# Halving the row scans at the start of an mLSTM and mixture-of-experts kernel

## The reference, cut to what matters

```python
for t in range(S):
    m_new = np.maximum(f_gate[:, :, t] + m, i_gate[:, :, t])
    f_stab = np.exp(f_gate[:, :, t] + m - m_new)
    i_stab = np.exp(i_gate[:, :, t] - m_new)
    m = m_new
    C = f_stab[..., None, None] * C + i_stab[..., None, None] * np.einsum('bhd,bhe->bhde', vt, kt)
    n = f_stab[:, :, None] * n + i_stab[:, :, None] * kt
    h_tilde = np.einsum('bhde,bhe->bhd', C, qt)
    denom = np.maximum(np.abs(np.einsum('bhd,bhd->bh', n, qt)[:, :, None]), 1.0)
    y[:, :, t] = sigmoid(o_gate[:, :, t]) * h_tilde / denom
```

## Time and profile before

| | us |
|---|---|
| median of 3 runs | 825.75 |
| lowest, highest | 824.54, 826.11 |
| the profiled execution | 824.76 |
| its span in the trace | 823.0 |
| first tile's exponent product starts | 17.80 |
| last product of the mixer starts | 177.29 |

### The profile page before, as it was taken

How to read it: one execution, slowest core, us unless ns; L and a number is a source line. 1 busy time by engine, 2 the same in 40 slices (tenths; PEclk the granted TensorE clock), 3 DMA queues, 4 the chain that set the end, 5 groups by cost and what they waited for, 6 DMA issues and landing times.

```text
span 823.0 us, 17685 instructions
## 1 busy us (share of the span) xinstructions
PE 782.3 (95%) x6036; PEld 726.4 (88%) x6036; DVE 521.2 (63%) x1424; ACT 468.7 (57%) x997; POOL 394.0 (48%) x467
## 2 busy tenths in 40 slices
PE   5899999989989999999999999999999999999994
PEld 4898898977878889999999989999998999999894
DVE  5566777767669667765865686487658657442431
ACT  5455545522427752884587287538826762892672
POOL 3545455454623752655166246507633651673233
PEclk9999999999999999999999999999999999999998
DMA  4999999714420312121121212112121212121000
GB/s 75 140 157 167 152 183 154 137 57 119 123 60 20 86 49 69 48 72 46 48 79 49 69 37 66 56 46 71 49 81 30 61 49 70 53 67 40 2 1 24
DMA packets 137987, 60.96 MB, mean 74 GB/s; under 512 B 104696, under 2 KB 136184, under 8 KB 137912
## 3 DMA queue, kind: packets, MB, share of 16 engines
q1 hardware_dynamic: 135608, 52.13, 29.8%
q0 software_dynamic: 2304, 7.87, 3.0%
HBM read 51.67 MB, written 8.26 MB: 73 GB/s over the span
## 4 chain that ended last, share of the span: by engine, by line
PE 63%; DVE 6%; ACT 5%; issue 2%; POOL 1%; DMA 0%; ACTq 0%; POOLq 0%
PE bank L1857 7%; PE bank L1942 7%; PE bank L1858 6%; PE bank L1860 6%; PE bank L1944 6%; PE bank L1943 6%; PE bank L1862 3%; PE bank L1861 3%; PE bank L1898 3%; PE bank L1900 3%; PE bank L1899 3%; PE bank L1794 2%; PE bank L1886 1%; PE bank L1883 1%; DVE unit L1535 1%
## 5 line engine op out<-in xcount | busy, mean ns | idle before, releaser
L1272 POOL TENSOR_TENSOR gl_lo<-unit,gl_hi 128x384 fp32r<-128x384 f32 x128 | 130.5, 1019 | 263.2 <-ACT gl_hi L1732 263.1
L1942 PE MATMUL bank<-Wo_hi,gl_hi 128*128 128x320 f32 x384 | 124.8, 325 | 0.5 <-POOL gl_lo L1272 0.5
L1944 PE MATMUL bank<-Wo_hi,gl_lo 128*128 128x320 f32 x384 | 118.6, 309 | 0.0
L1943 PE MATMUL bank<-Wo_lo,gl_hi 128*128 128x320 f32 x384 | 118.4, 308 | 0.0
L1532 DVE SCALAR_TENSOR_TENSOR unit<-bank,unit 128x384 f32<-128x384 f32 x104 | 57.8, 556 | 74.7 <-ACT bank L1725 74.7
L1696 ACT ACTIVATE hid_hi<-bank 128x384 fp32r<-128x384 f32 x64 | 31.5, 491 | 125.6 <-PE bank L1862 125.6
L1713 ACT ACTIVATE unit<-bank 128x384 f32<-128x384 f32 x128 | 62.3, 487 | 50.4 <-PE bank L1862 41.3
L1857 PE MATMUL bank<-x_hi,Wi_hi 128*128 128x384 f32 x224 | 80.2, 358 | 2.4 <-DVE unit L1535 1.6
L1858 PE MATMUL bank<-x_hi,Wi_lo 128*128 128x384 f32 x224 | 75.8, 338 | 0.0
L1942 PEld LDWEIGHTS bank<-Wo_hi,gl_hi 128*128 128x128 f32 x384 | 72.5, 189 | 3.1 <-POOL gl_lo L1272 3.1
L1535 DVE TENSOR_TENSOR unit<-unit,bank 128x384 f32<-128x384 f32 x128 | 70.9, 554 | 4.4
(11 more groups left out here) (296 smaller groups left out, 2084.0 us busy)
## 6 DMA issues: line engine op xcount, KB each, us to landing
stage<-in_moe_w_dram SPq DMA_DIRECT2D x32, 320.0 KB, 3.0
stage<-in_moe_w_dram SPq DMA_DIRECT2D x32, 256.0 KB, 2.6
stage<-in_moe_w_dram SPq DMA_DIRECT2D x96, 64.0 KB, 2.4
k_in<-in_k_dram SPq DMA_DIRECT2D x24, 160.0 KB, 3.8
q_in<-in_q_dram SPq DMA_DIRECT2D x24, 160.0 KB, 4.5
o_in<-in_o_gate_dram SPq DMA_DIRECT2D x24, 160.0 KB, 4.0
v_in<-in_v_dram SPq DMA_DIRECT2D x24, 160.0 KB, 3.6
x_rows<-xt SPq DMA_DIRECT2D x24, 160.0 KB, 3.2
```

Source lines behind the costliest of these rows:

```text
L1272: nc.gpsimd.tensor_tensor(gl_lo[:, b, :], ex[:, b, :], gl_hi[:, b, :].bitcast(F32), ALU.subtract).then_inc(gl_ok, 1)
L1942: nc.tensor.matmul(acc[j][:, 0:DM], gl_hi[:, f % RG, t_], Wo_hi[:, f, :], start=(f == 0), stop=False)
L1943: nc.tensor.matmul(acc[j][:, 0:DM], gl_hi[:, f % RG, t_], Wo_lo[:, f, :], start=False, stop=False)
L1944: ins = nc.tensor.matmul(acc[j][:, 0:DM], gl_lo[:, f % RG, t_], Wo_hi[:, f, :], start=False, stop=(f == NF2 - 1))
```

## The change

Five things are changed, all in the prologue and the first tiles.

1. The DVE steps on rows are done twice, for columns 0 to 383 (three chunks) and then for 384 to 767 (`rows_of(0)`, `rows_of(1)`). The second half's maximum starts from the first half's last column. The low parts of the second half are put off until after tile 0's product of scores and W (`low_parts(1)` in DVE's `body`).
2. PE's turning into columns and ACT's exponentials are done by halves as well: the first half before tile 0, the second half inside tile 1 (`columns_of_rows(1)` between `addend` and `products`, `by_token(1)` at the end of ACT's tile 1), in bank 7. PE, POOL and DVE wait for them (`cols_step` 6) where they first use chunk 3, or the bank. ACT's high parts of the second half come after tile 0's W.
3. SP's loads no longer wait for the pads: tile 0's k, q, o follow the gates at once, v waits for its own clearing, and k and q of tile 1 follow. Six loads are issued ahead of the exponents' rows. `part_rows` is written after the first weight piece, and `load_exponents(0, 1)` comes after tile 3's loads.
4. Two small DMAs (`first_rows` of the low parts) go from SP to ACT, and the three of `w_gate` go to GpSimd's queue.
5. POOL clears `exp_l[0]` and the v buffers first; ACT prepares its constants by halves; PE starts its constant products when `ident` is there, 21 of them instead of 18.

```diff
-            sp.wait_ge(const_ok, 3)
             load(0, 0, 0)
+            sp.wait_ge(values_zero, 1)
             load_values(0, 0, 0)
-            sp.wait_ge(exp_const, 1)
+            load_rows(0, 1, 1)
+            sp.wait_ge(exp_const, 2)
             sp.wait_ge(parts_hi, 1)
-            first_rows(0)
+            first_rows(sp, 0)
             sp.wait_ge(parts_hi, 2)
             first_columns(0)
-            sp.wait_ge(rows_step, 10)
-            first_rows(1)
-            sp.wait_ge(rows_step, 11)
+            sp.wait_ge(rows_step, C_LO)
             first_columns(1)
-            sp.dma_start(part_rows.rearrange("j r t -> r j t"), parts[:].bitcast(F32)).then_inc(parts_out, 16)
-            load(0, 1, 1)
+            load_out_gates(0, 1, 1)
+            sp.wait_ge(values_zero, 3)
             load_values(0, 1, 1)
-            for n, (a, w) in enumerate(XK):
-                sp.dma_start(wg[0:w, n, 0:E], w_gate[a:a + w, :]).then_inc(wg_in, 16)
             load(0, 2, 2)
             load_values(0, 2, 2)
-            sp.wait_ge(parts_out, 16)
-            load_exponents(0, 1)
...
             weights(0)
+            sp.wait_ge(rows_step, ALL_ROWS)
+            sp.dma_start(part_rows.rearrange("j r t -> r j t"), parts[:].bitcast(F32)).then_inc(parts_out, 16)
...
             for j in range(NCH - RING):
                 turn(j, (0, j), 0, RING + j, j % RING)
+                if j == 0:
+                    sp.wait_ge(exp_const, 4)
+                    sp.wait_ge(parts_out, 16)
+                    load_exponents(0, 1)
...
+            pool.wait_ge(wg_zero, 1)
+            for n, (a, w) in enumerate(XK):
+                nc.gpsimd.dma_start(wg[0:w, n, 0:E], w_gate[a:a + w, :]).then_inc(wg_in, 16)
...
+            def low_parts(half):
+                mine, first = slice(half * SPAN, (half + 1) * SPAN), half * HALF_STEPS
+                dve.wait_ge(parts_hi, 2 * half + 1)
+                row_step(nc.vector.tensor_tensor(parts[:, 1, mine], A_rows[:, mine], parts[:, 0, mine].bitcast(F32), ALU.subtract))
+                dve.wait_ge(rows_step, first + C_AT)
+                dve.wait_ge(parts_hi, 2 * half + 2)
+                row_step(nc.vector.tensor_tensor(parts[:, 3, mine], c_rows[:, mine], parts[:, 2, mine].bitcast(F32), ALU.subtract))
...
+            rows_of(0)
+            rows_of(1)
...
                 if last:
                     finish(*last)
+                if peeled(b) and b == 0 and c == 0:
+                    low_parts(1)
...
+            row_constants(0)
+            column_constants(0)
+            row_constants(1)
+            high_parts(0)
+            column_constants(1)
+            act.wait_ge(rows_step, A_LO)
+            first_rows(act, 1)
+            by_token(0)
...
                     nc.scalar.activation(W[u][:, par], pE[par], ACT.Exp).then_inc(w_ok, 1)
+                if peeled(b) and b == 0 and c == 0:
+                    high_parts(1)
...
+                if peeled(b) and b == 0 and c == 1:
+                    by_token(1)
...
-            pe.wait_ge(const_ok, 3)
-            warm(18)
-            pe.wait_ge(rows_step, 13)
...
+            pe.wait_ge(const_ok, 1)
+            warm(21)
+            columns_of_rows(0)
             warm(7)
             pe.wait_ge(cols_ok, 1)
             pe.wait_ge(cols_step, 3)
-            pe.wait_ge(exp_const, 1)
-            pe.wait_ge(pads_ok, 2 * RING)
+            pe.wait_ge(exp_const, 2)
+            pe.wait_ge(pads_ok, 2 * RING + 1)
...
                 if last:
                     carried(*last)
                     addend(*last)
+                if peeled(b) and b == 0 and c == 1:
+                    columns_of_rows(1)
                 if last:
                     products(*last)
```

More of the change, by code:

```diff
@@ L217, in peeled, with own_half, first_rows @@
             return isinstance(g, int)
+        FIRST_STEPS, HALF_STEPS = 3, 10
+        A_AT, C_AT, A_LO, C_LO = (FIRST_STEPS + n for n in (5, 6, 7, 8))
+        LAST_AT = FIRST_STEPS + 10, FIRST_STEPS + HALF_STEPS + 8
+        ALL_ROWS = FIRST_STEPS + 2 * HALF_STEPS
+        def own_half(b, c):
+            return peeled(b) and b == 0 and c == RING
         def three_beside(g, u):
             return u == RING - 1 and not (peeled(g) and g < RING)
+        def first_rows(eng, j):
+            for par in range(2):
+                row = par * DP + H + j
+                eng.dma_start(exp_r[0][row:row + 1, :, :].bitcast(F32),
+                              parts[par:H:2, j, 0:SPAN].bitcast(F32)).then_inc(exp_in[0], 16)
         @block.sync
@@ L342, in _ @@
                                         pattern=[[-1, NP]], channel_multiplier=1).then_inc(const_ok if n == 3 else pool_step, 1)
+            nc.gpsimd.memset(exp_l[0][:].bitcast(F32), 0.0).then_inc(exp_zero, 1)
+            for u in range(RING):
+                nc.gpsimd.memset(v_in[u][:], 0.0).then_inc(values_zero, 1)
             for u in range(RING):
@@ L364, in body @@
                 g, u, i = tile_of(b, c)
+                if own_half(b, c):
+                    pool.wait_ge(cols_step, 6)
                 if c < NCH - 1:
@@ L501, in body @@
                 last = before_it(b, c, 1)
+                if own_half(b, c):
+                    dve.wait_ge(cols_step, 6)
                 if last:
@@ L549, in _, with row_constants, column_constants @@
             act.wait_ge(const_ok, 2)
-            for half in range(2):
-                nc.scalar.copy(exp_r[half][:, :, :], head_sel[:, :].unsqueeze(2).broadcast_to([P, NP, SPAN]))
-            act.wait_ge(exp_zero, 2)
-            for half in range(2):
+            def row_constants(half):
+                nc.scalar.copy(exp_r[half][:, :, :], head_sel[:, :].unsqueeze(2).broadcast_to([P, NP, SPAN])).then_inc(exp_const, 1)
+            def column_constants(half):
+                act.wait_ge(exp_zero, half + 1)
                 for mine in HALVES:
@@ L565, in _ @@
-            nc.scalar.activation(eZ[:, :, :].rearrange("p (b c) h -> p b c h", b=B),
-                                 pcols[1].rearrange("p c (b h) -> p b c h", b=B), ACT.Exp)
-            for par in range(2):
-                rows = slice(par * 64, par * 64 + 64)
-                nc.scalar.activation(carry[rows, :, :].rearrange("p (b c) n -> p b c n", b=B),
-                                     plast[rows, :].rearrange("p (b n r c) -> p r b c n", b=B, r=2, c=NCH)[:, par],
-                                     ACT.Exp).then_inc(cols_step, 1)
+                ins.then_inc(exp_const, 1)
@@ new lines, in high_parts, with by_token @@
+            def high_parts(half):
+                mine, first = slice(half * SPAN, (half + 1) * SPAN), half * HALF_STEPS
+                act.wait_ge(rows_step, first + A_AT)
+                nc.scalar.copy(parts[:, 0, mine], A_rows[:, mine]).then_inc(parts_hi, 1)
+                act.wait_ge(rows_step, first + C_AT)
+                nc.scalar.copy(parts[:, 2, mine], c_rows[:, mine]).then_inc(parts_hi, 1)
+            def by_token(half):
+                chunks = slice(half * RING, (half + 1) * RING)
+                act.wait_ge(prepT, half + 1)
+                nc.scalar.activation(eA[:, :, :].rearrange("p (b c) h -> p b c h", b=B)[:, :, chunks],
+                                     pcols[half][0].rearrange("p (c b h) -> p b c h", b=B, h=H), ACT.Exp).then_inc(cols_step, 1)
+                nc.scalar.activation(eZ[:, :, :].rearrange("p (b c) h -> p b c h", b=B)[:, :, chunks],
+                                     pcols[half][1].rearrange("p (c b h) -> p b c h", b=B, h=H), ACT.Exp)
+                for par in range(2):
+                    rows = slice(par * 64, par * 64 + 64)
+                    nc.scalar.activation(carry[rows, :, :].rearrange("p (b c) n -> p b c n", b=B)[:, :, chunks],
+                                         plast[half][rows, :].rearrange("p (b n r c) -> p r b c n", b=B, r=2, c=RING)[:, par],
+                                         ACT.Exp).then_inc(cols_step, 1)
@@ L692, in carried @@
                     pe.wait_ge(fin_step, g * 6 - 4)
+                if peeled(g) and g == 1:
+                    pe.wait_ge(cols_step, 6)
                 pe.wait_ge(c_ok, states_through(b, c - 1))
```

111 lines of the change are left out of this document (55 added, 56 removed).

## The result

The changed kernel takes 821.82 us, median of 8 runs (820.15 to 824.64); the kernel before takes 826.25 in the same comparison. The ratio is 0.9944, 95% interval 0.9923 to 0.9965, so 4.6 us are won (4.4 by the two medians), and between 2.9 and 6.4. Forecast were 819.6 and 6.0 us. Two later comparisons of the same kernel gave 0.9903 (0.9868 to 0.9938) and 0.9928 (0.9895 to 0.996).

A forecast was written before the change was run, and what follows sets the result against it. PE bounds the steady run from tile 4, so time won before it is kept: 6.1 us by tile 2, less 1.2 for the clock, plus 1.1 at tile 3, is 6.0; 825.75 - 6.0 = 819.75, forecast 819.6, range 817.6 to 822.8.

The forecast's parts named there:

- The steady run decides, and keeps what is won ahead of it: Mixer from tile 4: PE busy 120.73 of 122.17 us, so each us won before should be won at the end.
- Tile 0 opens behind DVE's second half, at 14.3: Prologue: PE waits for DVE's row steps on both halves; opening at 14.3 against 17.80, bounds 13.7 and 15.2.
- Cover for the small DMAs, 1.6 us: Prologue: the last small exponent DMA lands at 12.7, 1.6 us before tile 0 opens.
- Moved DMAs cost and bring nothing: Prologue: DMAs on other queues save only issue time; no gain counted, gate-weight DMAs on POOL costed at nothing.
- Tiles 0 and 1 in 3.16 and 6.05: First tiles: tile 0 takes 3.16; tile 1 takes 4.8 plus 0.65 for second-half columns and 0.6 waiting for ACT.
- 1.2 for the clock: Tiles 0 and 1: one stretch of PE at half clock, charged 1.2 us, bounds 0 and 1.6.
- the forecast's case: Whole kernel: one half-clock stretch in tiles 0 and 1, 6.0 us gained, 818.8 to 820.8 us, chance 0.50.
- the rival of two or more stretches: Prologue: a second half-clock stretch costs another 1.2 to 1.6 us; part of a rival at 821 to 823, chance 0.22.
- Tile 3 loses its 1.10: Tile 3: its load is issued at 21 to 22 instead of 32.06, so its extra 1.10 us goes.
- The rest unchanged: After the first tiles: the steady pace and the experts stay as they were.
- gain lost later: Kernel's end: it waits for something not moving with the tiles, such as a DMA; within 1.6 of 825.75, chance 0.06.
- less is won: Prologue: two half-clock stretches, DVE at its upper bound, or exponents' rows behind six loads; 821 to 823 us, chance 0.22.

The follow-up runs named there:

- early loads alone: Kernel before, with tile 0's k, q, o loaded at once and tile 1's k and q issued ahead of the small DMAs; 824.15 us, ratio 0.9958.
- early clearing: Changed kernel with the two memsets PE waits for moved ahead, behind the third step of DVE's second half; 819.40 us, ratio 0.991 to before.
- more constant products: Changed kernel with 26 and 15 constant products instead of 21 and 7 around the first half's transposes; 819.84 us, ratio 0.9904 to before.
- both: Changed kernel with early clearing and 24 and 9 constant products, run twice; 819.35 and 819.32 us, ratios 0.9888 and 0.9894 to before.
- columns by GpSimd: Kernel of both, with the last two small exponent DMAs issued by GpSimd and 7 constant products before tile 0, not 9; 818.81 us, ratio 0.9882.

## Why the prediction was right, step by step

- **The steady run decides, and keeps what is won ahead of it.** Right. From tile 4 to the experts' start the changed kernel takes 135.39 us (173.87 - 38.48), before it took 136.08 (178.91 - 42.83). The 0.7 less was not forecast; all three profiles have it (135.38 to 135.42), and early loads alone doesn't (136.07). Its cause stays open. The mixer's last product starts at 172.25, 170.98 and 171.42, where 171.3 was forecast.
- **Tile 0 opens behind DVE's second half, at 14.3.** Right: 14.16, 14.19 and 14.49. A scan of 384 took 0.94 to 1.00 (0.95 was taken), a plain step 0.55 with a start to start of 0.47 to 0.58 (0.50), the diagonal 0.24 (0.35). The early clearing showed that this was the wait.
- **Cover for the small DMAs, 1.6 us.** They had landed by 13.02 or earlier, as the early clearing showed, so the cover was 1.1 us or a little more.
- **Moved DMAs cost and bring nothing.** Right for this kernel, by the run with all of them on SP. Behind the early clearing it is not: there two small DMAs moved from SP to GpSimd are issued by 10.83 instead of 11.65, and tile 0 opens 0.8 us sooner.
- **Tiles 0 and 1 in 3.16 and 6.05, and 1.2 for the clock.** The tiles at full clock take 3.15 and 6.44: the second was 0.4 short, by two errors. PE's own work was put at 5.45 and is 6.11, the wait for ACT at 0.6 and is 0.33. The clock is the term that was mis-sized: 1.2 us was charged, for one stretch, with bounds of 0 and 1.6. The first profile lost 2.6 us in three stretches. There the clock fell at 11.4, before the hole ahead of tile 0 had begun, while the prediction had it fall after that hole; PE had been idle from 7.92 to 9.35 as well, and that hole was not counted. Two other executions had the one stretch, in the place forecast (between 14 and 19), which cost 1.3 and 1.4 by the same sum, and tile 4 at 37.22 and 37.62, 5.6 and 5.2 us ahead, where 6.0 was forecast. So the forecast's case and the rival of two or more stretches both occur, from one execution of the same program to the next. The hole before the transposes isn't the same in them: 1.43 us in the first, 0.86 and 0.92 in the others, whose first constant products took longer (see the last section). Whether that decides is not shown.
- **Tile 3 loses its 1.10.** Right in all three: its load was issued at 22.50, it took 6.06.
- **The rest unchanged.** The work is, its time is not, for two reasons. The first is the clock. Behind tile 4, the last microseconds left out, the changed kernel's profiles had two stretches at half clock each, of 3.4 or 6.8 us, which cost 1.4 to 1.9 us each (the leads before and behind them). So had most other variants, near 168 to 181, 227 to 237, or 266 to 274, while three profiles (more constant products, early loads alone, and the second of both) had none. The kernel before had none there in its profile at a clock of 0.994, but its other 50 runs have a mean of 0.9904, so stretches are common there too.
- **The gain kept to the end.** Only in part, and this is the second reason. The prediction gave "gain lost later" 0.06 and thought of a DMA. What the trace shows are three short DVE steps in the experts' first token lists (`sel`, `mem`, `lo`) that end only with POOL's product beside them. Taken together they are over their shortest times (0.22, 0.24 and 0.18) by 0.6 us before, by 2.3, 2.0 and 2.2 in the changed kernel's profiles, by 1.2 with more constant products, 0.5 with the early clearing, 1.0 and 1.7 with both, and 0.1 with the columns by GpSimd. Winning time in the prologue shifts when the steps meet POOL's weight work, and in the changed kernel they meet it badly: 1.4 to 1.8 us of the gain are lost so, at full clock.
- **The size.** 4.6 us of 6.0. The median, 821.8, is in the range but past the forecast's own case (818.8 to 820.8), in that of "less is won", whose condition, two stretches or more, the first profile meets. That it came so near is in part luck: the losses behind the mixer were in no sum, nor was the 0.7 won in the steady run. At equal clock the changed kernel is 7.0 to 7.9 us ahead by the pooled fit (825.5 against 818.5, 818.1 and 817.6), and 5.8 to 6.7 with each kernel's own slope (0.76 before, 0.55 over the 21 runs of the changed one). By the profiles with one stretch in the prologue, as before has, it is 6.3 and 5.9 ahead at the mixer's end, and 1.4 and 1.6 less behind these DVE steps. The gap of 1 us and more between these accounts is not explained; there is only one profile of before, and its execution (824.8) was faster than the four other runs of that kernel at its clock (825.5 to 826.6).

## What to carry to other kernels

When a change shortens the way to a PE-bound run, count PE's holes on that way as well as its length. The clock can take back much of what the waits gave, and how much differs between executions of the same program. A few more constant products in the holes kept the clock up to tile 4 in all five profiles that had them, and cost 0.4 us at most; the early clearing, which shortens the hole, kept it alone in the one profile it has. Look also at what is released together with the last step: here two memsets of 0.1 us stood behind a half of the rows that tile 0 didn't need, and moving them was worth at least as much as the constant products. Then follow the lead past the stage that was changed: here 1.6 of 5.0 us went in the next stage, where two engines met at another moment than before. And an early load can be worth more for leaving its issuing queue free than for landing early.

## What the runs showed of the hardware

- PE's granted clock fell to 0.50 in the same program at different places from run to run, for 3.4 us or two or three times that; in the changed kernel's prologue 3.4 us in two profiles and 10.2 in one. Time against mean clock explains most of the spread: 0.67 us for 0.001, correlation within a kernel 0.73 to 0.98.
- The first batch of constant products, of the same instructions, took from 6.44 to 7.76 us in six executions (42 instructions), and 6.96 to 8.06 in four others (48 instructions). They start 0.22 us apart at first and 0.11 apart later, just twice as fast, and the change comes at another moment in each execution (4.6 us in the first profile of the changed kernel, 5.9 and 6.4 in the others). In the first:

```profile
3.00:4.50 1.50, 1.50 (x9) 1.50 (x9) 1.03 (x2) 1.49 (x3) 1.50 (x3) 1.00 1.02 173
4.60:6.00 1.40, 1.40 (x15) 1.40 (x14) 1.36 (x4) 1.38 (x2) 1.40 (x7) 1.00 1.42 170
```

  In all thirteen profiles the trace's own records of the clock begin at just that moment, so the 1.00 shown ahead of it is not a reading. Half the pace is what half clock would give; the trace doesn't record it.
- Three short DVE steps (128x8 to 128x24, 0.18 to 0.24 us) ran beside POOL's products of two tensors (1.3 to 1.6 us) in the first 60 us of the experts. In 22 of 39 cases, three steps in each of thirteen profiles, the DVE step ended 0.02 to 0.05 us behind the end of POOL's product, having taken up to 1.5 us. In the other 17 it took its shortest time.
- The three DMAs of the gate weights cost GpSimd 1.88 us of issue in the changed kernel and SP 3.33 before (20.81 to 24.14, in a queue full of loads), 1.66 with the queue emptier.
